# Seven block products in the second matrix product of an attention + FFN kernel as well

## The reference

```python
qn = q / (norm(q, axis=1) + 1e-6); kn = k / (norm(k, axis=1) + 1e-6)
s  = softmax(kn.transpose(0, 2, 1) @ qn / tau)          # [B, 256, 256]
x  = (v @ s).reshape(B * N, C)                          # 12032 tokens
h  = x @ w_in                                           # [12032, 2048]
out = (h * sigmoid(h)) @ w_out                          # silu, then [12032, 256]
```

## Time and profile before

| | |
|---|---|
| time, median of 3 runs | 1074.14 us (1074.05 to 1074.95) |
| span of the profiled execution, first to last instruction | 1072.1 us |
| busy in it: PE, PEld, DVE, ACT, POOL | 1067.7, 902.5, 730.0, 633.9, 62.0 us |
| TensorE's granted clock | 1.000 (of 2.4 GHz) over the whole span |

### The profile page before, as it was taken

The page is one execution under the profiler, slowest core; times in us unless marked ns, Lnnn a source line. Parts: engine busy times, 40 slices in busy tenths (PEclk is TensorE's granted clock), DMA queues, the critical chain, the costliest instruction groups (busy, mean ns, idle before and its releaser), DMA issues.

```text
span 1072.1 us, 13055 instructions
## 1 busy us (share of the span) xinstructions
PE 1067.7 (100%) x4848; PEld 902.5 (84%) x4848; DVE 730.0 (68%) x941; ACT 633.9 (59%) x789; POOL 62.0 (6%) x33
## 2 busy tenths in 40 slices
PE   9999999999999999999999999999999999999998
PEld 8988888888888888888999888888888888888998
DVE  6889787567566566566788776667567566566665
ACT  7998665555555555555666655555555555555554
POOL 3792000000000000000000000000000000000000
PEclk9999999999999999999999999999999999999999
DMA  9991000200200200200200200200200200200100
GB/s 358 397 362 40 1 1 1 79 1 1 79 1 0 78 0 0 73 0 0 79 1 1 74 1 1 79 1 1 79 1 1 78 0 0 73 0 0 40 1 35
DMA packets 26365, 54.08 MB, mean 50 GB/s; under 512 B 2512, under 2 KB 6864, under 8 KB 26320
## 3 DMA queue, kind: packets, MB, share of 16 engines
q1 hardware_dynamic: 25888, 52.86, 13.5%
q10 hardware_dynamic: 432, 0.62, 0.2%
HBM read 41.16 MB, written 12.32 MB: 50 GB/s over the span
## 4 chain that ended last, share of the span: by engine, by line
PE 99%; DMA 0%; SPq 0%; ACT 0%; issue 0%
PE ps_o L530 16%; PE ps_o L531 16%; PE ps_o L529 16%; PE ps_h L496 14%; PE ps_h L495 14%; PE ps_h L494 14%; PE ps_o L434 5%; PE ps_o L449 1%; PE ps_o L456 1%; DMA qk<-k_dram 0%; PE ps_h L486 0%; PE ps_h L488 0%; PE ps_h L487 0%; PE ps_o L487 0%; PE ps_o L486 0%; PE ps_o L488 0%
## 5 line engine op out<-in xcount | busy, mean ns | idle before, releaser
L496 PE MATMUL ps_h<-b_hi,a_lo_rest 128*128 128x512 f32 (+1 forms) x504 | 194.1, 385 | 0.0
L495 PE MATMUL ps_h<-b_lo,a_hi_rest 128*128 128x512 f32 (+1 forms) x504 | 194.1, 385 | 0.0
L494 PE MATMUL ps_h<-b_hi,a_hi_rest 128*128 128x512 f32 (+1 forms) x504 | 194.0, 385 | 0.0
L978 DVE TENSOR_TENSOR h_b<-ps_h,u 128x512 f32<-128x512 f32 x96 | 66.4, 692 | 162.2 <-PE ps_h L496 162.1
L956 DVE TENSOR_TENSOR u<-ps_h,u 128x512 f32<-128x512 f32 x96 | 66.4, 692 | 142.4 <-PE ps_h L496 91.2
L750 ACT ACTIVATE h_a<-ps_h 128x512 f32<-128x512 f32 x96 | 57.4, 598 | 162.6 <-PE ps_h L496 162.6
L530 PE MATMUL ps_o<-g_lo_a,wo_hi 128*128 128x512 f32 (+1 forms) x384 | 147.9, 385 | 0.0
L529 PE MATMUL ps_o<-g_hi_b,wo_hi 128*128 128x512 f32 (+1 forms) x384 | 147.9, 385 | 0.0
L531 PE MATMUL ps_o<-g_hi_b,wo_lo 128*128 128x512 f32 (+1 forms) x384 | 147.9, 385 | 0.0
L529 PE MATMUL ps_o<-g_hi_a,wo_hi 128*128 128x512 f32 (+1 forms) x384 | 147.9, 385 | 0.0
L530 PE MATMUL ps_o<-g_lo_b,wo_hi 128*128 128x512 f32 (+1 forms) x384 | 147.8, 385 | 0.0
(11 more groups left out here) (138 smaller groups left out, 1602.1 us busy)
## 6 DMA issues: line engine op xcount, KB each, us to landing
v_raw<-v_t_dram SPq DMA_DIRECT2D x40, 256.0 KB, 3.7
out_t_dram<-v_raw SPq DMA_DIRECT2D x20, 512.0 KB, 3.2
qk<-q_dram SPq DMA_DIRECT2D x17, 384.0 KB, 10.8
...
w_in_raw<-w_in_dram SPq DMA_DIRECT2D x4, 512.0 KB, 11.8
wo_raw<-w_out_dram SPq DMA_DIRECT2D x4, 512.0 KB, 12.3
```

Source lines behind the costliest of these rows:

```text
L494: nc.tensor.matmul(ps_h[:, bank, 0:n], w_hi, x_hi, start=start, stop=False, skip_group_check=True)
L495: nc.tensor.matmul(ps_h[:, bank, 0:n], w_hi, x_lo, start=False, stop=False, skip_group_check=True)
L496: return nc.tensor.matmul(ps_h[:, bank, 0:n], w_lo, x_hi, start=False, stop=stop, skip_group_check=True)
```

## The change

From step 1 on (n >= 8, `FIRST`) FFN2 is done with seven products too. For pair n the factors are `F1` to `F7`, made of the four 128x128 blocks of `w_out`, and the other side is g11, g12, g22, g21 and their sums: `t13_raw` (T1 and T3), `t2_raw` (T2), and T4, which takes the place of g21 in `h`. Their triples are called `f22`, `f11`, `f_t4`, `f_t3`, `f21`, `f_t1`, `f_t2`. Six of them are summed over the pairs of a step, each in a PSUM bank of its own (`m1`, `m3` to `m7`). The seventh, `f21`, has no bank left: it uses FFN1's bank Y, ACT copies it out for each pair (`flush`), and a DMA issued by POOL adds it to the output in DRAM (`add_flushed`). At a step's end ACT copies m3, m1, m7, m4, m5 (`copy_m3` ...), DVE joins them in pairs 2 to 4 of the next step (`sum_u`, `make_nv`, `sum_c22`), and stores and accumulating DMAs (`add_o7`, `add_o1`, `add_u`, `add_nv`) put them into the output.

FFN1 has two PSUM banks, X and Y, instead of four: products are added in PSUM where they can be, ACT first copies P1 from X to Y (`seed_u1`), and its order on PE is P1, P6, P2, P5, P7, P3, P4. The four results have an ACT and a DVE instruction of 512 columns each.

The factors: POOL makes them once from `w_out` (`part`, 8 of them) and DVE subtracts (`split_part`), during steps 0 and 1; they go to DRAM and come back for every pair into a ring of two (`load_ring_a`, 640 KB, and `load_ring_b`, 256 KB). The sums of x's blocks are made by accumulating DMAs from DRAM (`add_x`), and each of the seven blocks is rounded and subtracted by itself (`round_x`, `split_x`). The second batch's A is kept in DRAM and made again by POOL (`prepare_a1`) in pairs n = 40, 41, 43, ..., 53. Step 0 keeps the old FFN2 (`first_step`), in the new order. All loops are written out.

```diff
+            def load_ring_a(n):
+
+                if n < FIRST + PAIRS:
+                    sp.wait_ge(part_stored, part_stored_by(n - FIRST))
+                sp.wait_ge(used[H21], max(n - 1, PAIRS - 1))
+                sp.dma_start(ring[:, n % 2, :, 0:F5, :].bitcast(F32), s_dram[n % PAIRS, :, :, 0:F5, :]).then_inc(ring_a[n % 2], 16)
...
+            def begin_c21(it):
+                sp.wait_ge(o4_copied, it)
+                sp.dma_start(out_block(it, 1, 0), o4[:, 0:tokens_of(it)[1]]).then_inc(c21_begun, 16)
...
+                load_ring_a(n)
+                if it > 1 and pair == 0:
+                    begin_c12(it - 1)
+                if it > 1 and pair == 1:
+                    begin_c21(it - 1)
+                if it > 1 and pair == 4:
+                    store_c22(it - 1)
...
+                if pair == PAIRS - 1 and it + 2 < ALL:
+                    sp.wait_ge(x_split, 3 + FACTORS * it)
+                    load_x(it + 2)
+                load_ring_b(n)
...
+            def part(i):
+                raw, sums_, high = part_tiles(i)
+                a12, a22, a11, a21 = (raw[:, j, :] for j in range(4))
+                f7, f5, f6 = (sums_[:, j, :] for j in range(3))
+                pool.wait_ge(part_loaded, 32 * (i + 1))
...
+                pool.wait_ge(part_step, 3 * i + 3)
+                nc.gpsimd.tensor_copy(high[:, 0:4, :].bitcast(F32R), raw)
+                nc.gpsimd.tensor_copy(high[:, 4:7, :].bitcast(F32R), sums_).then_inc(part_rounded, 1)
...
+            def add_flushed(n):
...
+                    pool.wait_ge(fl_stored, 16 * flushed)
+                    nc.gpsimd.dma_start(out_block(it, 0, 0), fl[:, 0:tok], accum_op=ALU.add).then_inc(fl_stored, 16)
...
+            def add_o1(it):
+                pool.wait_ge(o1_copied, it)
+                pool.wait_ge(fl_stored, 128 * it)
+                nc.gpsimd.dma_start(out_block(it, 0, 0), o1[:, 0:tokens_of(it)[1]], accum_op=ALU.add).then_inc(
+                    o1_stored, 16)
+
+            def add_o7(it):
+                pool.wait_ge(o7_copied, it)
+                pool.wait_ge(c21_begun, 16 * it)
+                nc.gpsimd.dma_start(out_block(it, 1, 0), o7[:, 0:tokens_of(it)[1]], accum_op=ALU.add).then_inc(
+                    c21_stored, 16)
...
+            def prepare_a1(pair):
...
+                pool.wait_ge(p4_done, SWITCH + pair + 1)
+                nc.gpsimd.tensor_copy(a_hi(pair)[:, 0:3, :], a1_raw[:, 0:3, :])
+                nc.gpsimd.tensor_copy(a_hi(pair)[:, 3:7, :], sums[:]).then_inc(a1_rounded, 1)
...
+            for n in range(FIRST + 2, PERIODS):
+                it, pair = divmod(n, PAIRS)
+                if n - 2 <= PAIRS * FINAL - 1:
+                    add_flushed(n - 2)
+                if it > 1 and pair == 1:
+                    add_o7(it - 1)
+                    add_o1(it - 1)
+                if it > 1 and pair == 2:
+                    add_u(it - 1)
...
+            def p4(n, pair, par, tok):
+                pe.wait_ge(c22_made, n + 1)
+                product(pair, par, tok, BANK_Y, A22, T4, False).then_inc(p4_done, 1)
...
+            def second(n, factor, x_hi, x_lo, out, start, tok):
+                w_hi, w_lo = ring[:, n % 2, 0, factor, :], ring[:, n % 2, 1, factor, :]
+                nc.tensor.matmul(out[:, 0:tok], w_hi, x_hi[:, 0:tok], start=start, stop=False, skip_group_check=True)
...
+            def f_t2(n):
+                it, pair = divmod(n, PAIRS)
+                pe.wait_ge(t2_lo, n - FIRST + 1)
...
+                second(n, F6, g_hi[:, GT2], g_lo[:, GT2], m6, pair == 0, width(n)).then_inc(used_t2, 1)
...
+            def pair_step(n):
+                it, pair = divmod(n, PAIRS)
+                par, tok = it % 2, tokens_of(it)[1]
+                wait_for_step(n)
+                p1(n, pair, par, tok)
+                if n > FIRST + 1:
+                    f_t1(n - 2)
+                f22(n - 1)
+                p6(n, pair, par, tok)
+                p2(n, pair, par, tok)
+                f11(n - 1)
+                p5(n, pair, par, tok)
+                p7(n, pair, par, tok)
+                if n > FIRST + 1:
+                    f_t2(n - 2)
+                p3(n, pair, par, tok)
+                p4(n, pair, par, tok)
+                f_t4(n - 1)
+                f_t3(n - 1)
                 pe.wait_ge(c21_made, n + 1)
...
+                f21(n - 1)
...
+            def closing_products(n):
+                f_t1(n - 1)
+                f22(n)
+                f_t2(n - 1)
+                f11(n)
+                f_t1(n)
+                f_t2(n)
+                f_t3(n)
+                pe.wait_ge(fl_added, PAIRS - 2)
+                f21(n)
+                f_t4(n)
...
+            def seed_u1(n, tok):
+
+                act.wait_ge(p1_done, n + 1)
...
+                nc.scalar.activation(ps_h[:, BANK_Y, 0:tok], ps_h[:, BANK_X, 0:tok], ACT.Copy).then_inc(u1_seeded, 1)
...
+            def round_t2(n, tok):
+                act.wait_ge(t2_made, n - FIRST + 1)
+                if n > FIRST:
+                    act.wait_ge(used_t2, n - FIRST)
+                else:
+                    act.wait_ge(used[H12], FIRST)
+                nc.scalar.activation(g_hi[:, GT2, 0:tok], t2_raw[:, 0:tok], ACT.Copy).then_inc(t2_hi, 1)
...
+            ROUND_X = {2: (B11, B21), 3: (B22,), 4: (T2,), 5: (T1,), 6: (T3,), 7: (T4,)}
+
+            def pair_step(n):
+                it, pair = divmod(n, PAIRS)
+                tok, before = width(n), width(n - 1)
+                if FIRST <= n - 2 <= PAIRS * FINAL:
+                    flush(n - 2)
+                round_h(n - 1, before, H21, silu_21)
+                seed_u1(n, tok)
+                if n == FIRST + 1:
+                    copy_out(0, 1)
+                round_t13(n - 1, before)
+                if it > 1 and pair == 1:
+                    copy_m7(it - 1)
+                copy_u(n, tok)
+                round_t4(n - 1, before)
+                silu_c11(n, tok)
+                round_h(n, tok, H11, silu_11)
+                copy_w(n, tok)
+                if it > 1 and pair == 0:
+                    copy_m3(it - 1)
+                    copy_m1(it - 1)
+                if it > 1 and pair == 1:
+                    copy_m4(it - 1)
+                    copy_m5(it - 1)
+                if it < FINAL:
+                    for block_ in ROUND_X.get(pair, ()):
+                        round_x(it + 1, block_, block_)
+                round_t2(n - 1, before)
+                silu_c22(n, tok)
+                silu_c12(n, tok)
+                round_h(n, tok, H22, silu_22)
+                silu_c21(n, tok)
...
+            SPLIT_X = {3: (B11,), 4: (B21,), 5: (B22, T2), 6: (T1, T3), 7: (T4,)}
...
+            def make_c22(n, tok):
+                dve.wait_ge(p7_done, n + 1)
+                dve.wait_ge(w_copied, n + 1)
...
+                nc.vector.tensor_tensor(h[:, H22, 0:tok], ps_h[:, BANK_Y, 0:tok], w[:, 0:tok], ALU.add).then_inc(
+                    c22_made, 1)
...
+            def sum_u(it):
+
+                tok = tokens_of(it)[1]
+                dve.wait_ge(used_t2, PAIRS * it)
+                dve.wait_ge(o1_stored, 16 * it)
+                nc.vector.tensor_tensor(o1[:, 0:tok], m6[:, 0:tok], o1[:, 0:tok], ALU.add).then_inc(u_summed, 1)
...
+            PARTS_AT = {2: (0, 1), 3: (2,), 4: (3,), 6: (4,), 8: (5,), 10: (6,), 12: (7,)}
...
+                split_h(n, TOK, H22)
+                if n == 0:
+                    split_wo(PARTS - 1)
+                for i in PARTS_AT.get(n, ()):
+                    split_part(i)
+                make_c21(n, TOK)
+                split_h(n, TOK, H12)
+                if n < PAIRS - 2:
+                    sum_a(0, n + 2)
...
+            def pair_step(n):
+                it, pair = divmod(n, PAIRS)
+                tok, before = width(n), width(n - 1)
+                if n - 2 > PAIRS * FINAL:
+                    add_flush(n - 2)
+                sum_t2(n - 1, before)
+                split_h(n - 1, before, H21)
+                if it > 1 and pair == 2:
+                    sum_u(it - 1)
+                if it > 1 and pair == 3:
+                    make_nv(it - 1)
+                if it > 1 and pair == 4:
+                    sum_c22(it - 1)
+                sum_t4(n - 1, before)
+                split_t13(n - 1, before)
+                split_t4(n - 1, before)
+                if it < FINAL:
+                    for block_ in SPLIT_X.get(pair, ()):
+                        split_x(it + 1, block_, block_)
+                split_h(n, tok, H11)
+                make_c22(n, tok)
+                split_t2(n - 1, before)
+                make_c21(n, tok)
+                for i in PARTS_AT.get(n, ()):
+                    split_part(i)
+                if n - 1 in reload_at:
+                    split_a1(reload_at[n - 1])
+                sum_t13(n, tok)
+                split_h(n, tok, H22)
+
+            def closing(n):
+                tok = width(n)
+                add_flush(n - 1)
```

(55 more changed lines are left out.)

1113 lines of the change are left out of this document (754 added, 359 removed).

## The result

The changed kernel takes **1188.44 us** (median of 4 runs, 1185.15 to 1190.02) against 1074.18 of the kernel before on the same chip: a ratio of 1.106, 95% interval 1.104 to 1.108. That is slower, as forecast, but by 114 us instead of 15, and outside the range. The profiled execution has a span of 1183.3 us, where the sum said 1086.6.

The account below looks back on a forecast made before the run. PE bounds the kernel: fewer triples give a 1017.2 us span including 12.5 at the end; waits of 28.0 + 7.7 + 16 + 5.4 + 2.5 + 4.8 + 5 make 1086.6, plus 2.0 for the median: 1089 us, range 1052 to 1122.

Parts of the forecast that it names:

- (c): Pair 2 of ten steps: `sum_u` waits for o1's addition in DRAM, stall S - 2.26 with S the landing; 16 us, bounds 0 and 47.
- rival 2: The accumulating DMA is slow, 7.4 us to land, making (c) 46 us and the time 1119; chance 0.11.
- (a): Pairs 6 and 7: DVE's `split_x` waits for ACT's `round_x` ahead of `make_c22`, holding P4 1.4 us each; 28.0 us.
- (b): Work ahead of `make_c22` in pair 5 (0.47) and pairs 3 and 4 (0.11), `copy_m7` in pair 1 (0.1); 7.7 us.
- Rival 1: P4 isn't held in pairs 6 and 7, so (a) is nothing and the time is 1061, faster; chance 0.25.
- rival 4: ACT paces the pair at 9.9 us without overlap, 32 us in place of (a) to (c); time 1064, chance 0.07.
- (f): POOL's tensor work and DVE exclude each other; 0.45 us for each of 11 blocks, 5 us, bounds 0 and 39.
- (d): Step 0: `split_part` ahead of `make_c21` and H12's remainder, plus ACT's rounds of x; 5.4 us.
- turn: Change to the new order at n = 8 and 9: four copies out, no filler in pair 9; 2.5 us, between 0 and 5.
- (e): `split_a1` and parts at n = 8, 10, 12 behind `make_c21` make H22's remainder late for slot 2; 0.44 x 11 = 4.8 us.
- Hidden work: Ring loads, flush, loads of x and the SP and POOL issues are covered by PE's work and cost nothing.
- Rival 3: o1's addition lands like a store, 2.0 us, so (c) is 0 and the time 1073, no change; chance 0.12.

Follow-up runs that it names:

- e7: The changed kernel with every GpSimd output DMA a plain store instead of an accumulating one, additions in DRAM left out; 1148.16 us, ratio 1.069.
- e8: The changed kernel without the ring's factor loads after the first two pairs, so products use stale factors; 1162.78 us, ratio 1.082.
- e4: The changed kernel with only POOL's queue order altered: `add_o1` issued before `add_o7`; 1121.13 us, ratio 1.044.
- e1: The changed kernel with `sum_u` writing to a buffer of its own, so DVE no longer waits for o1's addition in DRAM; 1122.44 us, ratio 1.046.
- e2: The changed kernel with only DVE's order altered: a pair's last `split_x` stands behind `make_c22` instead of ahead; 1154.35 us, ratio 1.075.
- e9: e6 with factor block 3 back ahead of `make_c21` in pair 4 and block 1 back in pair 2; 1068.41 us, ratio 0.9954.
- e5: The changed kernel with e1, e2 and e4, two buffers each for flush and reloaded weights, two reloaded blocks one pair later; 1076.96 us, ratio 1.003.
- e6: e5 with step 0's splits and x rounding later in a pair, factor block 1 and step 2's x rounding one pair later; 1073.62 us, ratio 1.000.
- e10: e9 with GpSimd's eight operations per reloaded weight block on two columns instead of 128; 1060.07 us, ratio 0.988.

## Why the prediction was wrong, and where it was right

**The step that failed is (c), by its landing of 4.4 us.** Its mechanism and formula held: o4's store landed in 2.04 us (2.2 in the sum), POOL issued `add_o7` 8.98 us into pair 1 (8.7) and `add_o1` 0.54 later (0.4). With a landing of 8.24 the moment S is 8.1 us into pair 2, and the stall by S - 2.26 is 5.9; PE was idle for 5.70. But the landing was taken as 4.4, two plain stores' worth, since the DMA queues of the trace before were nearly empty. As the price of an addition that is first in the queue 4.4 was good (o7's took 4.1). The change fills the queues itself: o7's addition just ahead of o1's, and 896 KB of factors for every pair, 640 of them issued at the start of the very pair. e7, e8 and e4 show that the addition, what stands beside it and its place all count. With 8.24 the formula gives 59 us for ten steps. The rest had no term at all: the sum took a stall at its length, and PE came out of it at half the clock, 1.7 us more each time. So even rival 2, with 7.4, was too cheap at 46 us. By e1 the term is 66 us, against 16 in the sum and 47 as its upper bound.

**(a) held.** Pair 7 of step 2 (timeline of the changed kernel):

```profile
374.12 0.62 ACT L1129 ACTIVATE b_hi<-x_raw 128x512 fp32r<-128x512 f32 x1
...
374.78 0.69 DVE L1507 TENSOR_TENSOR b_lo<-x_raw,b_hi 128x512 fp32r<-128x512 f32 x1 [1.47 <-ACT b_hi L1129]
...
375.39 0.69 DVE L1546 TENSOR_TENSOR g_lo<-h,g_hi 128x512 fp32r<-128x512 f32 x1
...
375.99 0.68 DVE L1532 TENSOR_TENSOR h<-ps_h,w 128x512 f32<-128x512 f32 x1
...
376.73 0.50 PE L802 MATMUL ps_h<-b_hi,a_hi_last 128*128 128x512 f32 x1 [1.16 <-DVE h L1532]
```

Round, split, H11's remainder, c22, P4: the pair is 11.06 (10.92 in the sum). e2 gives back 34.1 us, where (a) and pair 5's share of (b) were 28.0 + 4.7. Rival 1 falls. So does rival 4: the pairs in which nothing is put ahead of `make_c22` take 9.6, not 9.9 (its sum had left out the 5 us of (f), too). **(b)** held: pair 5 is 10.11, 0.51 over the base (0.47), pairs 1, 3 and 4 are 9.7 (0.1 over).

**The base pair** is 9.60, not 9.52: 0.08 in each pair, 7 us over the 87 of them. It is not the reserve at P4: in pair 0 of step 2 PE's starts there are 0.23 apart like the others, and the excess is spread in hundredths over several products. Its cause is open.

**(d) was too small.** Step 0 lost 15.0 us against 5.4. POOL's sums for the factors took up to 1.47 us each beside DVE, so that in pair 2 DVE reached the second block's split 2.0 us before it was ready, with c21 and H12's remainder behind it. Moving these splits and ACT's rounding of x (e9) brought back 7.4 us against e5, in one profile each; pairs 0 and 1 are each 1.3 longer in every variant, which I did not price. **Pair 2 of step 1** had no term at all. I wrote that x's loads have a step; this one is issued only after step 0's output has left the same buffer, at 224.60, and ACT's `round_x` waited for it, 7.3 us with the low clock behind it. e6 moved the round and the pair was 10.0. The **turn** (2.5) held: pairs 8 and 9 together are 20.06, 1.7 over the 18.4 of their 27 triples.

**(e) and (f)** were 9.8 us for 11 blocks. Outside pair 2, steps 5 and 6 lost some 12 us for the 8 blocks in them. GpSimd's own operations are 8.1 us of these two steps in e10 (pair 2 included). The lock is real, and the choice of 0.45 us a block was half of the 1.0 measured; taken to its end, the rule of the Trainium skill (SBUF — State Buffer, section "SBUF: two separate sides") would have charged 30 us for these eight, an estimate from the 3.8 us of GpSimd a block in the sum. **Hidden work:** the ring was in time in steady pairs, as said, but not in pair 2 of step 5, where SP stood behind `load_a1`'s wait. I had counted SP's issues and not its waits. In that step the same wait also held the store of o4, with which o1's chain begins, so pair 2 took 21.7. Pair 2 of steps 5 and 6 is still 11 us too long in e1, which is most of the difference between pair 2's 79 us in the profile and e1's 66.

**The end** took 14.4 us from the last pair's end instead of 12.5, and the opening is 2.8 longer in the profile (first seed at 100.93 instead of 98.15). How much of that is the change's is open: with the same opening the first seed comes at 98.33 to 100.80 in the profiles of the other runs.

The span's miss of 96.7 us comes apart by the profile as: pair 2 of steps 2 to 11, 79 instead of 16, 63; step 0, 10; the base pair, 7; pair 2 of step 1, 6.5; steps 5 and 6 without pair 2, 5; the opening, 3; the end, 2; pairs 3 to 5 of step 1, 1.5; the turn, -1. That is 97. The sign was right with 0.58 put on slower, but the forecast of 1089 was far out. The forecast's own range of 1077 to 1105 also does not follow from its rule: (c) and (f) between half and double give 1078.5 to 1110, which changes nothing here.

**Rival 3** was a landing like a store's, with an estimate of 2.6 us by the figures of the Trainium skill (DMA: Bandwidth & Descriptors, section "Anatomy of one DMA — SWDGE (gpsimd) path"). The trace doesn't agree for additions: none of o1's landed in under 5.5, and none into the output in under 3.6. As plain stores, o7's in e7 land in 2.3 (median), which is near it.
